# A mixture-of-experts chain on one core: the third batch's rows also reach the first expert tile by products with 0/1 matrices, and the scatters of rows are moved

## What is computed

```python
# attention: batch 4, 8 heads, 576 positions, head width 64
q_d, k_d, v_d = means over 4 neighbouring positions          # 144 positions
out = repeat(softmax(q_d k_d^T / 8) v_d, 4) + softmax(where(|i-j| < 4, q k^T / 8, -1e9)) v
x = out.transpose(0, 2, 1, 3).reshape(2304, 512)              # one row for each token
# top-1 mixture of 8 experts
expert = argmax(normalised x @ normalised emb.T / tau);  gate = its softmax weight
y[mask] = gate * (relu(x[mask] @ w1[e]) @ w2[e])              # w1 512x1024, w2 1024x512
# dense block
h = y @ w_in;  out = maximum(0.01 h, h) @ w_out               # 512x2048, 2048x512
```

## Time and profile before

| | |
|---|---|
| Runs (us) | 895.75, 893.05, 896.04; median 895.75 |
| Profiled execution | 895.6 us, span 893.9 us |
| PE busy | 873.4 us, 98% of the span |
| DVE, ACT, POOL busy | 539.6, 513.4, 189.6 us |
| Chain that ended last | PE 89%, DVE 3%, ACT 2%, POOL 2%, issue 2% |
| Attention and first tile | 0 to about 166 us |
| Experts, dense block | to 893.9 us |

### The profile page before, as it was taken

One profiled execution on the slowest core, in us unless ns is written; L12 is line 12 of the kernel. 1 busy time (PEld: TensorE's weight loads), 2 busy tenths in 40 slices (PEclk: granted clock), 3 DMA queues, 4 the chain that ended last, 5 costly groups with the idle time before them and its releaser, 6 DMA issues.

```text
span 893.9 us, 16168 instructions
## 1 busy us (share of the span) xinstructions
PE 873.4 (98%) x5865; PEld 739.7 (83%) x5868; DVE 539.6 (60%) x781; ACT 513.4 (57%) x912; POOL 189.6 (21%) x279
## 2 busy tenths in 40 slices
PE   8999998999999999999999999999999999999997
PEld 5888876777787778777878988998998998998996
DVE  5677756898999999999886553223223224224222
ACT  4778866888888888888885443223223223223222
POOL 7677874400010022520001002002002002001000
PEclk8999969999999999999999999999999999999999
DMA  7587684665467285531101002002001001000000
GB/s 215 160 254 225 198 271 175 209 234 213 145 246 285 86 308 129 216 73 50 37 24 48 1 1 72 1 1 70 0 0 61 10 0 45 25 0 33 4 1 36
DMA packets 44946, 92.94 MB, mean 104 GB/s; under 512 B 4632, under 2 KB 23944, under 8 KB 40784
## 3 DMA queue, kind: packets, MB, share of 16 engines
q1 hardware_dynamic: 34752, 43.95, 16.3%
q0 software_dynamic: 9952, 47.81, 15.0%
q10 hardware_dynamic: 176, 0.31, 0.2%
HBM read 72.97 MB, written 19.09 MB: 103 GB/s over the span
## 4 chain that ended last, share of the span: by engine, by line
PE 89%; DVE 3%; ACT 2%; POOL 2%; issue 2%; DMA 0%; another core or an unknown queue 0%; ACTq 0%; DVEq 0%; POOLq 0%; SPq 0%
PE banks L988 73%; PE banks L920 3%; PE banks L1034 2%; PE banks L898 2%; PE banks L862 2%; PE banks L809 1%; PE banks L892 1%; PE banks L995 1%; DVE elo L1625 1%; PE banks L874 1%; PE banks L817 1%; PE banks L1053 1%; ACT ehi L1266 1%; DVE flo L1713 0%; DVE fg L1708 0%
## 5 line engine op out<-in xcount | busy, mean ns | idle before, releaser
L1625 DVE TENSOR_TENSOR elo<-wslot,ehi 128x1024 fp32r<-128x1024 f32 x196 | 239.3, 1226 | 26.9 <-ACT ehi L1266 16.2
L1266 ACT ACTIVATE ehi<-wslot 128x1024 fp32r (+1 forms) x196 | 207.4, 1061 | 35.8 <-PE banks L988 32.2
L1708 DVE SCALAR_TENSOR_TENSOR fg<-fraw 128x384 f32<-128x384 f32 x96 | 53.6, 558 | 212.5 <-ACT fraw L1363 203.2
L1363 ACT ACTIVATE fraw<-banks 128x384 f32<-128x384 f32 x96 | 47.2, 492 | 228.5 <-PE banks L988 225.3
L988 PE MATMUL banks<-zhi,winhi 128*128 (+1 forms) x384 | 130.7, 340 | 0.2 <-DVE winlo L1643 0.2
L988 PE MATMUL banks<-zhi,winlo 128*128 (+1 forms) x384 | 129.4, 337 | 0.0
L988 PE MATMUL banks<-zlo,winhi 128*128 (+1 forms) x384 | 129.0, 336 | 0.0
L988 PE MATMUL banks<-wouthi,fhi 128*128 128x512 f32 x288 | 113.1, 393 | 2.9 <-DVE flo L1713 2.9
L988 PE MATMUL banks<-wouthi,flo 128*128 128x512 f32 x288 | 114.0, 396 | 0.0
L988 PE MATMUL banks<-woutlo,fhi 128*128 128x512 f32 x288 | 113.6, 394 | 0.0
L988 PE MATMUL banks<-ehi,xThi 128*128 128x512 f32 x200 | 82.7, 414 | 3.2 <-DVE xTlo L1630 3.2
(11 more groups left out here) (221 smaller groups left out, 1448.6 us busy)
## 6 DMA issues: line engine op xcount, KB each, us to landing
wslot<-in_w POOLq DMA_DIRECT2D x24, 1024.0 KB, 6.4
wslot<-in_w SPq DMA_DIRECT2D x8, 1024.0 KB
xr<-xs SPq DMA_DIRECT2D x25, 272.0 KB
ys<-y_sb SPq DMA_DIRECT2D x25, 256.0 KB
qb<-in_qT SPq DMA_DIRECT2D x16, 288.0 KB, 4.1
vq<-in_vtok SPq DMA_DIRECT2D x32, 144.0 KB
kb<-in_kT SPq DMA_DIRECT2D x15, 288.0 KB, 4.8
vwin<-in_vtok SPq DMA_DIRECT2D x16, 245.0 KB
```

Of the source, the lines that this page charges most:

```text
L1266: act.activation(ehi[:, ring_at(k), :], wslot[:, chunk_cols(offs[dt], matrix, half, c)], ACT.Copy).then_inc(s_ehi, 1)
L1363: act.activation(fraw[:, f % 2, :], banks[:, f % 2, 0:TB], ACT.Copy).then_inc(s_fhev, 1)
L1625: dve.tensor_tensor(elo[:, ring_at(k), :], wslot[:, chunk_cols(offs[dt], matrix, half, c)], ehi[:, ring_at(k), :].bitcast(F32), ALU.subtra ...
L1708: dve.scalar_tensor_tensor(out=fg[:, f % 2, :], in0=fraw[:, f % 2, :], scalar=0.01, in1=fraw[:, f % 2, :], op0=ALU.mult, op1=ALU.max).then ...
```

## The change

- POOL's scatters of batches 0 and 1 are given by a table `SCATTER_AT`: two in step 10, one each in steps 11 to 14 (the last after the outputs of pair 12). The remaining three of batch 1 and all of batch 2 come after the outputs of the last pair.
- SP loads tile 0 after batches 0 and 1 only. POOL scatters batch 2 after that load has landed. Batch 2's rows get to tile 0 by 16 more products (4 blocks of 4 column blocks) with 4 more `hot` matrices, which DVE makes in step 18. They stand before `ranks` of batch 3, where 12 warm products were; 3 are left.
- SP waits for both batches' scatters before it loads tile 1. In the first tile `turn_x` of tile 1 stands behind the first half of `project`.
- `ranks` of batch 2 comes at the end of step 16. `add_v` of pair 14 comes behind the reciprocal. Four warm products are added in step 0.

```diff
-            return banks[:, 0, :] if k and g >= DRAIN else XROW
+            return banks[:, 1, :] if k and g >= DRAIN else XROW
...
+        SCATTER_AT = {10: (0, 0, 2), 11: (0, 2, 1), 12: (0, 3, 1), 13: (1, 0, 1), 14: (1, 1, 1)}
...
-            for b in range(B - 1):
+            for b in range(B - 2):
                 sp.wait_ge(s_scat[b], 16 * (TILES[b][1] - TILES[b][0]))
             sp.wait_ge(s_o6, NPAIR)
             sp.dma_start(xr[:, 0, :], xs[0:P, :]).then_inc(s_xl[0], 16)
...
-            sp.wait_ge(s_scat[B - 1], 16 * (TILES[B - 1][1] - TILES[B - 1][0]))
+            for b in (B - 2, B - 1):
+                sp.wait_ge(s_scat[b], 16 * (TILES[b][1] - TILES[b][0]))
...
-                if s >= 10 and (s - 10) // NP_ < B - 2:
-                    b, k = divmod(s - 10, NP_)
+                if s in SCATTER_AT:
+                    b, k, n = SCATTER_AT[s]
                     if k == 0:
                         indices(b)
-                        scatter(b, 0, TILES[b][1] - TILES[b][0] - NP_ + 1)
-                    else:
-                        scatter(b, TILES[b][1] - TILES[b][0] - NP_ + k, 1)
+                    if s == NPAIR - 2:
+                        gp.wait_ge(s_o6, NPAIR - 3)
+                    scatter(b, k, n)
...
+            gp.wait_ge(s_o6, NPAIR)
+            scatter(B - 3, 2, 3)
             indices(B - 2)
-            scatter(B - 2, 0, TILES[B - 2][1] - TILES[B - 2][0])
+            gp.wait_ge(s_xl[0], 16)
+            scatter(B - 2, 0, N2)
             indices(B - 1)
-            gp.wait_ge(s_xl[0], 16)
             scatter(B - 1, 0, MT)
...
                 if s == 0:
                     turn_emb()
+                    warm(4, 4)
...
-            warm(3, 1)
+            warm(3, 4)
             turn_rows(NPAIR - 1, 0)
             turn_rows(NPAIR - 1, 1)
-            warm(12, 3)
+            def gather_rows(b, j, at, first):
+                for c in range(KC):
+                    pe.matmul(banks[:, XB, c * P:(c + 1) * P], x_sb[:, (TILES[b][0] + j) % SLOTX, c, 0:P],
+                              hot[:, at, :], start=(first and c == 0), stop=False)
+            pe.wait_ge(s_hot, 1)
+            for j in range(N2):
+                gather_rows(B - 2, j, MT + j, j == 0)
+            warm(3, 3)
             ranks(B - 1, NPAIR - 1)
...
-                if not last:
+                if t and not last:
                     turn_x(t + 1, at)
                 project(t, 0, chunk_no(t, HC), ring_at(HC))
+                if not t:
+                    turn_x(t + 1, at)
                 turn_h(t, 1)
...
-                if g:
+                if 0 < g < NPAIR - 1:
                     add_v(g - 1)
...
+                if s == NPAIR + 2:
+                    hot_rows(B - 2, MT, ((0, N2),))
```

More of the change, by code:

```diff
@@ L130, in build @@
         KB_AT = QB_AT + 3 * S * 4
-        hot = at("hot", [NQ, MT, P], F32, QB_AT)
+        hot = at("hot", [NQ, MT + TILES[B - 2][1] - TILES[B - 2][0], P], F32, QB_AT)
         slot_no_i = at("slot_no_i", [NQ, P], I32, KB_AT)
@@ L379, in pairs @@
             return x[:, :, 0], x[:, :, 1]
+        N2 = TILES[B - 2][1] - TILES[B - 2][0]
+        SCATTER_AT = {10: (0, 0, 2), 11: (0, 2, 1), 12: (0, 3, 1), 13: (1, 0, 1), 14: (1, 1, 1)}
         QUARTER_AT = (4, 7, 10, 13)
@@ L733, in _ @@
                     gp.wait_ge(s_ss, NTOK)
+                    for b in (B - 2, B - 1):
+                        gp.wait_ge(s_scat[b], 16 * (TILES[b][1] - TILES[b][0]))
                 f0, f1 = NF * (e - SLOTS) // (E - SLOTS), NF * (e - SLOTS + 1) // (E - SLOTS)
@@ L964, in _ @@
                     outputs(s - 3)
-                if s == NPAIR:
-                    ranks(B - 2, NPAIR - 1)
                 if 0 <= s - 2 < NPAIR:
@@ L972, in _ @@
                     turn_rows(s - 4, 1)
-                if s >= 8 and (s - 8) % NP_ == 0 and (s - 8) // NP_ < B - 2:
-                    ranks((s - 8) // NP_, s)
-            warm(3, 1)
+                if s >= 8 and (s - 8) % NP_ == 0 and (s - 8) // NP_ < B - 1:
+                    ranks((s - 8) // NP_, min(s, NPAIR - 1))
+            warm(3, 4)
             turn_rows(NPAIR - 1, 0)
             turn_rows(NPAIR - 1, 1)
-            warm(12, 3)
+            XB, YB, HTB, HID = 0, 1, (2, 5), (3, 4)
+            def gather_rows(b, j, at, first):
[6 more added lines that the diff above has]
+            warm(3, 3)
             ranks(B - 1, NPAIR - 1)
             warm(5, 3)
-            XB, YB, HTB, HID = 0, 1, (2, 5), (3, 4)
             def split_product(dst, lhs, rhs, start, stop):
@@ L1001, in gather_x @@
                     if j in (0, 2):
-                        pe.wait_ge(s_hot, 1 if j == 0 else 2)
-                    for c in range(KC):
-                        pe.matmul(banks[:, XB, c * P:(c + 1) * P], x_sb[:, (TILES[B - 1][0] + j) % SLOTX, c, 0:P],
-                                  hot[:, j, :], start=(j == 0 and c == 0), stop=False)
+                        pe.wait_ge(s_hot, 2 if j == 0 else 3)
+                    gather_rows(B - 1, j, j, False)
                 pe.wait_ge(s_xl[0], 16)
@@ L1510, in choose, with hot_rows @@
                     .then_inc(s_oh, 1)
+            def hot_rows(b, at, parts):
+                t0 = TILES[b][0]
+                dve.wait_ge(s_pos, b + 1)
+                dve.wait_ge(s_slot_no, 1)
+                for a, z in parts:
+                    dve.tensor_tensor(hot[:, at + a:at + z, :], slot_no[:].unsqueeze(1).broadcast_to([NQ, z - a, P]),
+                                      pos[:, t0 + a:t0 + z].unsqueeze(2).broadcast_to([NQ, z - a, P]),
+                                      ALU.is_equal).then_inc(s_hot, 1)
             def place(b):
@@ L1524, in place @@
                 if b == B - 1:
-                    dve.wait_ge(s_pos, B)
-                    dve.wait_ge(s_slot_no, 1)
-                    for a, z in ((0, 2), (2, MT)):
-                        dve.tensor_tensor(hot[:, a:z, :], slot_no[:].unsqueeze(1).broadcast_to([NQ, z - a, P]),
-                                          pos[:, t0 + a:t0 + z].unsqueeze(2).broadcast_to([NQ, z - a, P]),
-                                          ALU.is_equal).then_inc(s_hot, 1)
+                    hot_rows(b, 0, ((0, 2), (2, MT)))
                     link(dve.tensor_tensor(early[:], EARLY, run[:], ALU.add))
@@ L1540, in _ @@
                     sums(s - 1)
+                    add_v(s - 2)
                 if s >= 8 and (s - 8) % NP_ == 0 and (s - 8) // NP_ < B - 1:
```

## The result

| | before | changed |
|---|---|---|
| median (20 executions each, same chip) | 894.67 us | 896.97 us |
| lowest to highest | 892.96 to 897.72 | 894.57 to 901.97 |
| ratio | | 1.0032 (95%: 1.0017 to 1.0046) |
| profiled execution | 895.6 (span 893.9) | 902.0 (span 900.2) |

The forecast was 892.6, three microseconds less. The time rose by 2.3. The profiled execution of the changed kernel is the slowest of its 20, so more traces were taken. Of all executions in this document one, of 1061.7 us in e13_before, counts as slow; it is left out of that run's ratio.

What follows compares the result with a forecast made beforehand. PE, busy 98% of the span, was taken as the bound, with time to gain only where it waits or runs at the lower clock. −8.1 + 0.6 − 1.5 + 1.8 + 1.0 + 3.2 = −3.0 from 895.6: 892.6 us, range 887.3 to 899.0.

Steps and rivals of the forecast that it cites:

- part 1: Drain of the attention: moving scatters away from the outputs removes late signals and the clock's fall, −8.1 us.
- part 2: Step 10: a second scatter makes POOL issue for 1.27 us more, so `normalise` starts later, +0.6 us.
- part 6: PE's wait for tile 1's rows, set by POOL's queue of scatters behind the last outputs, +3.2 us.
- part 4: 16 gather products of batch 2 and 3 warm ones ahead of `ranks`, +1.8 us; swapping `ranks` and `add_v` costs nothing.
- Rival B: Drain: scatters are not what holds the outputs up, so no gain there; +5.1 us, 900.7 us, chance 0.13.
- Part 3: Step 0: four warm products fit in PE's wait and keep the clock up from 9.4 to 16.3 us, −1.5 us.
- Parts 4 to 6: Behind the drain: gather products +1.8 us, `turn_x` of tile 1 behind `project` +1.0, wait for tile 1's rows +3.2.
- the mark: Instant when SP issues tile 0's load, the last pair's outputs being done: 139.88 us before, forecast at about 130.9.
- Part 7: Later loads: expert 1's w-quarters issued up to 7 us later, and bank 1 for bank 0, cost nothing.
- A: Tile 1's rows come in time, with a wait of 0 to 0.5 us: −6.2 us, 889.4 us, chance 0.30.
- C: The clock falls again in the wait for tile 1's rows: +3.4 us, 896.0 us, chance 0.15.
- D: DVE's six subtractions block POOL's scatters whole, 7.2 us in place of 3.0: +4.2 us, 896.8 us, chance 0.07.

Runs made afterwards that it cites:

- e13_before: The kernel before, unchanged, run again on the third chip for a second trace: median 891.0 us, ratio 0.9994, span 888.6.
- e3: The kernel before with only the four warm products in step 0 added: median 894.1 us, ratio 0.9999 to the kernel before.
- e4: The kernel before with batch 0's four scatters issued 2, 1, 1 in steps 10 to 12: median 896.0 us, ratio 1.0017 to the kernel before.
- e8: The kernel before plus a plain 256 KB DMA behind step 10's scatter: median 890.5 us, ratio 0.9998 to the kernel before.
- e11: The kernel before with only the new order in steps 16 and 17, its bank and the warm products: median 886.3 us, ratio 0.9944 to the kernel before.
- e6: The kernel before with warm products, single scatters and batch 2 scattered behind the last outputs, no products for it: 896.0 us, ratio 1.0062 to the kernel before.
- e12: The changed kernel with only the ranks of batch 2 back ahead of turn_second in step 16: median 897.6 us, ratio 1.0069 to the kernel before.
- e7: The changed kernel with 16 warm products ahead of turn_x of tile 1: median 892.6 us, ratio 1.0024 to the kernel before.
- e9: The changed kernel, unchanged, run again on the third chip: median 894.4 us, ratio 1.0035 to the kernel before, span 892.8.
- e1: The changed kernel, unchanged, run again on the first chip: median 896.5 us, ratio 1.0018 to the kernel before, span 895.4.
- e15: The kernel before with the new order in steps 16 and 17 but without the four warm products: median 886.4 us, ratio 0.9944 to the kernel before.
- e2: The changed kernel with one scatter in each of steps 10 to 14 and four behind the last outputs: 895.1 us, ratio 1.0007 to the kernel before.
- e16: The kernel before with the new order, warm products and step 14's pair of scatters split: median 886.5 us, ratio 0.9970 to the kernel before.

## Why the prediction was wrong, part by part

Three steps failed, and not the same ones on every chip: part 1's −8.1 where the drain had less to give, part 2's +0.6 where the new pair of scatters held PE, and the clock behind the wait of part 6, which the forecast put at nothing.

**Part 1, scatters away from the outputs (−8.1): its size holds where signals come late, and on the two later chips both size and cause are wrong.** The trace at hand gave −8.0. In five traces the drain with `ranks` at its old place took 30.0 (before), 29.0 and 28.4 (e3, e4, with late signals), 26.2 and 26.9 (e8, e13, without any). Against the changed kernel's 22.0 the gain is 6.4 to 8.0 where signals come late, and 4.2 and 4.9 where they don't. There the scatters had next to no part in it: e11 leaves them where they were and its drain takes 22.3, e6 scatters singly with `ranks` at its old place and needs 26.8 on the second chip, and e12 has them where the change puts them and needs 25.4. The step that failed is the last sentence of part 4, "That `ranks` of batch 2 and `add_v` change places costs nothing". It costs nothing, but it brought 3 to 5 us, and I did not ask what stood behind `ranks` in PE's queue. Rival B, which says that scatters are not what holds the outputs, had the cause right for those chips and the result wrong, since it let the whole gain go. How the 6.4 to 8.0 us divide between late signals and the order is not known: no kernel with the new order and the old scatters, or the reverse, ran on the first chip.

**Part 2, the second scatter in step 10 (+0.6): right where signals come on time, wrong where they don't.** Where the signal comes on time the stage costs 0.7 to 1.3 more (e7, e9, e12). In the traces where it comes late it cost +7.7, +3.1 and +1.4 (after, e1, e4): the two scatters in a row did there what I had blamed them for in the drain. I argued in part 1 that pairs of scatters hold PE's signals, and in part 2 costed a new pair by POOL's time alone.

**Part 3, warm products (−1.5): −1.5 in the trace, nothing in the medians** (e3, e15). It priced a stretch that three of the five traces without the warm products don't have.

**Parts 4 to 6 (+1.8, +1.0, +3.2): right.** Pair 15 to x of tile 1 was to take 6.0 more and takes 6.1 in both pairs of traces, 7.1 in e1. SP's load of tile 0 was issued at 144.15, nine scatters began at 147.56, 9.6 behind the mark (8.7 expected), and PE waited 3.0 to 3.7 us for tile 1's rows in the three traces. The scatters and the indices between them end at 161.47, 23.5 behind the mark (23.8 expected); three of the nine scatters are longer than the rest, by 2.5 us together (3.0 expected).

```profile
144.15 0.35 SPq L477 DMA_DIRECT2D xr<-xs  x1
...
147.56 1.82 POOL L596 DMA_INDIRECT xs<-x_sb,pidx  x1 [5.54 <-DMA xr<-xs]
149.69 1.95 POOL L596 DMA_INDIRECT xs<-x_sb,pidx  x1 [0.30 <-issue]
151.94 0.97 POOL L596 DMA_INDIRECT xs<-x_sb,pidx  x1 [0.30 <-issue]
...
158.58 1.61 POOL L596 DMA_INDIRECT xs<-x_sb,pidx  x1 [0.30 <-issue]
160.50 0.97 POOL L596 DMA_INDIRECT xs<-x_sb,pidx  x1 [0.30 <-issue]
...
167.45 0.66 PE L1010 MATMUL banks<-ident,xr 128*128 128x128 f32 x4 [3.18 <-DMA xr<-xs]
```

**Part 7: right.** From tile 2 to the end nothing changed (717.3 to 717.5 us).

**The rivals.** A did not occur: the wait was there. C occurred in all three traces of the changed kernel, for 1.1 to 2.2 us in place of 3.4; I gave it 0.15 because "the work on both sides of the wait is dense", and that does not protect. D did not occur: it adds 7.2 us to the scatters where 2.5 were added, and the stage took 6.1 us more where D has 10.2.

**The sum, with what was measured** in the pair e13 and e9: +0.5 to pair 8, +0.7 for the pair of scatters, −4.9 in the drain, +6.1 behind it, +1.8 of clock, together +4.2, the difference of the spans; the medians of that chip differ by 3.1. There the gain set against the tail was read from an execution, on another chip, that had more to lose.

Against the trace that I predicted from, e1 has −1.6 to pair 8, +3.1 for the pair of scatters, −8.0 in the drain, +7.1 behind it and +1.2 of clock; with −0.2 in the rest that is +1.5 where the forecast has −3.0. So where signals come late the drain gave what was forecast, and the sign turned on part 2 (2.5 us short), the clock (1.2) and the tail (1.1). In the changed kernel's first trace part 2 alone was 7.1 us short.

## What to carry to other kernels

Before a stall is priced from one profile, ask whether the stage takes the same in a second execution: here the drain took 30.0 us in one trace of the kernel before and 26.9 in another, on another chip, and that difference is as large as the forecast. For each instruction that an edit moves on an in-order engine, name what stood behind it and no longer waits. On the chip where the parts were taken apart, the small reordering was the whole gain (−5.1 us by itself), and the large move of scatters off the critical stage only put their cost where nothing hid it.

## What the hardware showed that I had not expected

PE's signals came late beside two scatters issued 1.3 us apart, and PE or ACT stood idle for 0.7 to 3.2 us each time. The waits of e4 from 112 to 139 us:

```profile
ACT od_sb L1185 <- remote: 4.4, 2, 3.0
PEld banks L880 <- remote: 2.5, 3, 1.3
...
PE banks L880 <- remote: 1.5, 2, 0.8
```

Of the first six traces, the five that have such pairs in front of the last outputs show it (before, after, e1, e3, e4), and e2, which has none, doesn't. Of the twelve later traces, on two other chips, none has a wait put down to "remote" between 80 and 140 us, and nine of them have pairs there. On those two chips the kernel before is 3 us faster. And in the first six traces no such wait stands beside the rows of three to nine scatters behind the last outputs. So the pairs seem needed for it and are not enough. What else differs was not found; the weight loads in flight beside them, for one, were not varied.

DVE's small subtraction of the choice (128x32, two inputs from SBUF) took 1.02 us beside POOL's 1.34 us product in e13. In e11, where POOL issued a scatter and then made the product, it took 1.79:

```profile
119.48 1.79 DVE L1510 TENSOR_TENSOR cand<-L_all,lmax 128x32 f32<-128x32 f32 x1
...
119.85 1.36 POOL L573 TENSOR_TENSOR pin<-pin,rs 128x700 f32<-128x700 f32 x1
```

For the last batch, with 40 columns and no product of POOL beside it, the same operation takes 0.20 in the changed kernel at 141.78. In e13 and e11 it ends with POOL's product. That is some 0.8 us of the 2.71 that PE waited for the choice in e13. The Trainium skill (SBUF — State Buffer, section "Who interferes with whom") says that a DVE instruction with two SBUF inputs and a GpSimd instruction that reads SBUF contend for ports that one of them holds exclusively. The rows of e13 agree; in e11 the subtraction began 0.4 us ahead of the product and still ended with it.

How long the granted clock stays at its lower level behind a wait differs between traces: behind the wait in step 10 it was 13.7 us, 3.4 us and not at all (after, e1, e4, with waits of 1.73, 0.69 and 0.68 us). Behind the wait for tile 1's rows it fell in all eight traces where PE stood idle there for 2.4 us or more, and not where the wait was filled (e7) or where it was 1.2 us (e11, e16).
